# Attention and two expert layers on one core: ScalarE and VectorE handle transposed blocks before exponentials and masked minima

## What is computed

```python
scores = scale * np.matmul(q, k.transpose(0, 1, 3, 2))
cum = np.cumsum(np.log(np.clip(f, 0.0001, 1.0)), axis=-1)
scores = np.where(causal, -1e9, scores + cum[:, :, :, None] - cum[:, :, None, :])
attn = np.exp(scores - scores.max(-1, keepdims=True))
attn = attn / (attn.sum(-1, keepdims=True) + 1e-09)
x = np.matmul(attn, v)              # -> (2304 tokens, 512)
h = x @ w_in                        # 512 -> 2048
g = np.where(h >= 1, h, np.where(h <= -1, 0.0, (h + 1) ** 2 / 4))
y = g @ w_out                       # 2048 -> 512
# then: each token to one of 8 experts by a softmax over cosine similarities, relu(y @ w1[e]) @ w2[e] * gate
```

## Time and profile before

| what | value |
|---|---|
| median of 3 runs | 963.71 us (963.3 to 965.04) |
| the profiled execution's own time | 962.55 us |
| its span | 960.8 us |
| TensorE matmul busy | 867.5 us (90%) |
| VectorE busy | 416.0 us (43%) |
| ScalarE busy | 404.8 us (42%) |
| GpSimd busy | 292.6 us (30%) |
| mean granted TensorE clock | 0.955 of full speed |

### The profile page before, as it was taken

The page is one execution under the profiler, slowest core; times in us unless marked ns, Lnnn a source line. Parts: engine busy times, 40 slices in busy tenths (PEclk is TensorE's granted clock), DMA queues, the critical chain, the costliest instruction groups (busy, mean ns, idle before and its releaser), DMA issues.

```text
span 960.8 us, 15119 instructions
## 1 busy us (share of the span) xinstructions
PE 867.5 (90%) x5106; PEld 806.4 (84%) x5107; DVE 416.0 (43%) x998; ACT 404.8 (42%) x924; POOL 292.6 (30%) x285
## 2 busy tenths in 40 slices
PE   5999999998899999999999999996299999999563
PEld 4788888888899999999999999996299889989231
DVE  3777788875554545444444444334511011101000
ACT  4777777775664344344345344335112112111010
POOL 8666777744675012012012011006200100110000
PEclk9999999999998999999999999997599999999787
DMA  5666777742010210210210320105580322001500
GB/s 187 189 206 202 229 232 231 226 124 65 25 50 25 91 50 26 91 50 25 91 50 26 112 72 7 60 1 176 146 261 24 97 88 75 35 33 33 203 29 4
DMA packets 66302, 94.82 MB, mean 99 GB/s; under 512 B 6598, under 2 KB 42438, under 8 KB 66192
## 3 DMA queue, kind: packets, MB, share of 16 engines
q1 hardware_dynamic: 58160, 79.43, 26.5%
q10 hardware_dynamic: 6336, 9.44, 2.7%
q0 software_dynamic: 1696, 4.72, 1.3%
HBM read 69.82 MB, written 24.27 MB: 98 GB/s over the span
## 4 chain that ended last, share of the span: by engine, by line
PE 80%; DVE 6%; ACT 5%; issue 3%; DMA 2%; SPq 1%; POOL 1%; DVEq 1%; POOLq 0%; ACTq 0%
PE psum L1303 19%; PE psum L1304 19%; PE psum L1305 19%; PE psum L1237 5%; PE psum L1278 5%; PE psum L1262 4%; PE psum L1446 2%; DVE ptl L942 1%; PE psum L1243 1%; ACT pth L743 1%; PE psum L1358 1%; PE psum L1357 1%; DVE g L971 1%; ACT xo L749 1%; PE psum L1430 1%
## 5 line engine op out<-in xcount | busy, mean ns | idle before, releaser
L1303 PE MATMUL psum<-xh,winh 128*128 128x384 f32 x384 | 132.5, 345 | 8.5 <-POOL winl L598 8.5
L1305 PE MATMUL psum<-xh,winl 128*128 128x384 f32 x384 | 131.0, 341 | 0.0
L1304 PE MATMUL psum<-xl,winh 128*128 128x384 f32 x384 | 130.8, 341 | 0.0
L1303 PE MATMUL psum<-gh,wouth 128*128 128x384 f32 x384 | 129.8, 338 | 0.0
L1304 PE MATMUL psum<-gl,wouth 128*128 128x384 f32 x384 | 129.6, 337 | 0.0
L1305 PE MATMUL psum<-gh,woutl 128*128 128x384 f32 x384 | 129.4, 337 | 0.0
L780 ACT ACTIVATE hpos<-psum,minus 128x384 f32<-128x384 f32 x96 | 55.8, 582 | 165.2 <-DVE hclip L968 164.9
L971 DVE TENSOR_TENSOR g<-hpos,hsq 128x384 f32<-128x384 f32 x96 | 62.3, 649 | 112.0 <-ACT hsq L782 112.0
L734 ACT ACTIVATE pr<-pr,mmin 128x64 f32<-128x64 f32 (+2 forms) x144 | 81.7, 567 | 39.9 <-DVE mmin L926 39.9
L1184 DVE SCALAR_TENSOR_TENSOR hl<-psum,hh 128x384 fp32r<-128x384 f32 x48 | 26.8, 557 | 161.7 <-ACT hh L862 161.7
L942 DVE TENSOR_TENSOR ptl<-psum,pth 128x512 fp32r<-128x512 f32 (+2 forms) x128 | 69.0, 570 | 38.2 <-ACT pth L743 37.8
(11 more groups left out here) (204 smaller groups left out, 1927.6 us busy)
## 6 DMA issues: line engine op xcount, KB each, us to landing
qraw<-q SPq DMA_DIRECT2D x16, 576.0 KB, 4.8
vraw<-vk SPq DMA_DIRECT2D x16, 320.0 KB, 2.9
kraw<-k SPq DMA_DIRECT2D x16, 288.0 KB, 3.6
c<-cum_d SPq DMA_DIRECT2D x32, 144.0 KB, 4.0
xa_d<-xo SPq DMA_DIRECT2D x16, 288.0 KB, 3.6
xb_d<-xo SPq DMA_DIRECT2D x16, 288.0 KB, 4.1
xst<-xa_d SPq DMA_DIRECT2D x24, 192.0 KB, 2.4
xst<-xb_d SPq DMA_DIRECT2D x24, 192.0 KB, 2.5
```

The lines of the kernel that those rows point to most:

```text
L1303: nc.tensor.matmul(psum_at, ah, bh, start=start, stop=False)
L1304: nc.tensor.matmul(psum_at, ah, bl, start=False, stop=False)
L1305: return nc.tensor.matmul(psum_at, al, bh, start=False, stop=stop)
```

## The change

In each step of attention's loop, ScalarE's `exp` moves behind its `high` copies, and VectorE's `masked` moves behind its `low` subtractions (and behind the copy of the turned denominators). No instruction is added or taken away, and all waits stay as they are. TensorE, GpSimd and SyncE keep their code.

```diff
@@ ScalarE
             for n in range(-AHEAD, STEPS + 1):
-                if 0 <= n + 2 < STEPS:
-                    exp(n + 2)
                 p, i = tile_of(n - 1)
                 if 0 <= n - 1 < STEPS:
                     for k in fills_of(i):
                         high(p, k)
+                if 0 <= n + 2 < STEPS:
+                    exp(n + 2)
                 p, i = tile_of(n)
                 if i == 7 and 0 <= p < PAIRS:
                     copy_early(p)
@@ VectorE
             for n in range(-AHEAD, STEPS + TAIL):
-                if 0 <= n + 3 < STEPS:
-                    masked(n + 3)
                 p, i = tile_of(n - 1)
                 if 0 <= n - 1 < STEPS:
                     for k in fills_of(i):
                         low(p, k)
                     if i == 8 and p >= 1:
                         copy_turned(p - 1)
+                if 0 <= n + 3 < STEPS:
+                    masked(n + 3)
                 p, i = tile_of(n)
                 if i == 7 and 0 <= p < PAIRS:
                     denominator(p)
```

## The result

The changed kernel is slower: 970.79 us median (968.95 to 971.34, 4 runs) against 963.5 us of the kernel before beside it, a ratio of 1.0074 with a 95% interval of 1.005 to 1.0099, which is +4.8 to +9.5 us. I had forecast +4.1 us and a time of 967.8, with a range up to 970.6. The direction was right, the size was too small by almost half, and the time lies just above the range.

What follows compares the result with a forecast made beforehand. TensorE was taken as the bound, stalling 0.66 us a pair before fill 6. 15 x 0.28 - 0.14 = about +4.1 us on 963.71 gave 967.8, own range 966.0 to 969.4, with rivals 964.8 to 970.6.

Steps and rivals of the forecast that it cites:

- TensorE is the bound, with 0.66 us of stall in one place per pair: In attention, TensorE paces each pair and idles 0.66 us before fill 6's first transpose, waiting for low 4.
- exp 1' and masked 2' out of the loop: Between turn 4 and turn 6, removing these from in front of high 4 and low 4 wins 0.
- masked 0' late: Behind low 3, masked 0' delays exp 0', copy_early and high 4, so fill 6 starts 0.28 us later in 15 pairs.
- The last pair: With no next pair, exp 8 no longer stands before high 2, so the change wins 0.14 us there.
- What else is later: Later masked and exp elsewhere cost 0: 0.2 us cover before attend_early; split_x in four pairs bounded by 0 to +0.1 each.
- The denominators and GpSimd's lock: VectorE's denominator, moved to 76.34, still falls into GpSimd's split of k and ends at the same time.
- rival 3: Denominator ahead of low 4 is caught by GpSimd's split of q: 0.17 x 15 = 2.6 us more, 970.4; 7 in 100.
- The sum: Whole kernel: 15 x 0.28 - 0.14 = +4.06 us, about +4.1, giving a median of 967.8 us.
- the first pair's +0.6: In attention's first pair, the same 0.28 us was taken, bounded by -0.3 and +0.6.

Runs made afterwards that it cites:

- Experiment 8: Changed kernel with masked 0' early, split_x two steps later, tile 2' scored behind turn 5, copy_early behind high 5: 958.53 us against 961.86 of the kernel before.
- experiment 1: Kernel before with only ScalarE's half of the change (high before exp): 962.16 us against 961.62, ratio 1.0006.
- experiment 3: Changed kernel with masked of a tile 0 kept ahead of low 2 and low 3: 967.84 us, ratio 1.0067 to the kernel before.
- experiment 6: Changed kernel with GpSimd's low part of q made by two instructions instead of one: 966.01 us, ratio 1.0044 to the kernel before.
- experiment 2: Kernel before with only VectorE's half of the change (low before masked): 996.57 us against 961.62, ratio 1.036.
- experiment 4: Changed kernel with both halves of split_x moved from the step of tile 1 to tile 3: 965.85 us, ratio 1.0045 to the kernel before.

## Why the prediction was right or wrong, point by point

- **TensorE is the bound, with 0.66 us of stall in one place per pair.** Right. Experiment 8 filled part of it.
- **exp 1' and masked 2' out of the loop: 0.** Right. In experiment 1 nothing stands between `copy_early` and `high 4`, in experiment 3 masked 2' is out of the way as well, and pairs stay at 12.67 to 12.70 us. The reading that decided it was the distance of 0.04 us between the end of the transposes and `high 4`, against the chain of waits; experiment 8 confirms it with ScalarE idle.
- **masked 0' late: 0.28 us in each of 15 pairs.** Right, with 0.25 measured. The place, the direct succession of exp 0', `copy_early` and `high 4`, and the stall (0.91 for 0.94) are as forecast; experiment 3 takes the loss away by moving this one call back.
- **The last pair: -0.14 us.** Right: 12.06 us instead of 12.18 from its predecessor's `low 4` to its own, -0.12. In experiment 1 it is 12.07, so it comes from ScalarE's half, as forecast.
- **What else is later: 0 for attend_early; 0 to 0.1 us in each of the four pairs with split_x.** This is the step that failed, by its second half. The cover for `attend_early` held. For the four pairs the prediction has only that the split "pushes `high 1` by perhaps 0.1": it follows the order on the queues, gives VectorE's `split_x` the duration that it had, and looks for a wait only at `attend_early`, not at the score of tile 8. ScalarE's half stands behind exp 3', as before; exp 3' waits for masked 3', and masked 3' now comes behind `low 6` and `low 7`. So VectorE's half comes 1.34 us later against GpSimd's queue (1.06 behind the start of the long instruction instead of 0.28 ahead of it), and the prediction did not look at what GpSimd runs by then. It had GpSimd as busy for 8.07 of 12.7 us, a row of an ordinary pair; in pair 7 it is busy for 10.46 of 12.69. The term was 1.14 us a pair (14.07 - 12.93), 4.6 us in all, where I had 0 and a bound of 0.4.
- **The denominators and GpSimd's lock.** The denominators did stay within the same instruction of GpSimd (VectorE reached `low 4` with 0.93 to spare), so rival 3 did not come. Its mechanism did, at another instruction of the same queue. That its 970.4 us lies so near to the measured 970.8 is chance: it was made of 15 x 0.17 us at the denominators, and nothing was lost there.
- **The sum.** 15 x 0.25 + 4 x 1.14 - 0.12 = 8.2 us, inside the measured 4.8 to 9.5; the first pair's 0.25 is taken from the others. (In the runs beside the experiments the kernel before had a median of 961.6 to 961.9.) The term that I left out, 4.6 us, is larger than the whole forecast of 4.1 us. What the profiled execution shows apart from that: attention's first pair is early (last section), so hidden unit 0 of the dense layer starts only 6.98 us later (228.41 for 221.43). The span has grown by 7.8; the other 0.8 us come in stages whose code is the same, and stay unexplained. The forecast's own range was also added up too narrowly at the top: 15 x 0.38 with the first pair's +0.6 gives about 970, not 969.4. That does not bring in the 4.6.

## What to carry to other kernels

When an instruction moves, price it by the neighbours that it has in its new place on the other engines, not by its old duration: VectorE's subtraction of two SBUF tensors took 0.56 us here when GpSimd stood still, and otherwise what was left of the GpSimd instruction that it came into, plus 0.41. That made 0.74 us near the end of one instruction and 2.04 early in the next, and a shift of 1.34 us lay between them. And of two engines in one pipeline, changing the order on one can be free and on the other dear: 0 us for ScalarE's alone, +35 for VectorE's alone, +7 for both. One producer that opens the next round, masked 0' here, has to keep its early place.

## What the runs showed of the hardware that I had not expected

VectorE and GpSimd wait for each other in both directions, and the turn changes at the boundary between two instructions. Wherever inside a GpSimd instruction VectorE's subtraction began, it ended 0.41 or 0.42 us after the end of that instruction: so it is in all 29 cases of `split_x` in attention, over the ten kernels, that met one, those of the kernel before (0.74 us) included. In the other 11 it took 0.56 us. GpSimd's next instruction was there at once in the kernel before and in experiment 6, but did not get ahead of VectorE: it took 3.01 us instead of 2.68, and 1.62 instead of 1.31.

TensorE gets fast at a time of its own during the first pair. Lines of one instruction, the mask's matmul, in the kernel before and then in the changed one; the columns are count, shortest/median/longest in ns, and first and last start:

```profile
L1247 PE MATMUL psum<-mask_b,ident_b x7: 263/277/277, 12.6 to 19.0; 128*128 128x64 bf16 x7
```

```profile
L1247 PE MATMUL psum<-mask_b,ident_b x5: 263/277/277, 12.7 to 16.2; 128*128 128x64 bf16 x5
L1247 PE MATMUL psum<-mask_b,ident_b x7: 202/203/207, 17.4 to 23.8; 128*128 128x64 bf16 x7
```

It still takes 277 ns at 19.0 us before, and 203 from 17.4 us in the changed kernel. The granted clock stands at 1.00 for the whole stretch from 12 to 24 us in both profiles, so this difference shows in the durations alone. With it, `low 4` of the first pair comes at 25.70 us instead of 26.68. Over the profiles of all these kernels but that of experiment 2 this `low 4` lies between 25.65 (experiment 4) and 27.10 us (experiment 6), and these two have the same order on ScalarE and VectorE up to there; GpSimd's low part of q is in one piece in the first and in two in the other, and what that adds is not shown. A single profile can be off by about a microsecond in its first pair, and distances between pairs are the better measure. Within a kernel, those of ordinary pairs behind the first repeat to 0.03 us.
